# Two groups of small matmuls split by batch half over the rows of the array

## The reference

```python
state = np.zeros((B, H, D, D))                      # B, H, S, D = 4, 8, 768, 40
for t in range(S):
    y[:, :, t] = np.einsum('bhd,bhde->bhe', rt, state)
    Sa = np.einsum('bhde,bhe->bhd', state, at)
    state_decay = state * wt[:, :, None, :] - np.einsum('bhd,bhe->bhde', Sa, bt)
    state = state_decay + np.einsum('bhd,bhe->bhde', vt, kt)
...
h = x @ w_in                                        # then SoLU, layer norm, @ w_out
g = np.maximum(h, 0.0) + alpha * np.minimum(h, 0.0) # with h = x @ w_in of the second layer; then @ w_out
```

## Time and profile before

| | us |
|---|---|
| median of 3 runs | 997.64 |
| lowest and highest run | 991.07 and 1005.46 |
| the profiled execution's own time | 1002.32 |
| its span in the trace | 1000.5 |
| mean granted clock of TensorE in it | 0.974 |

### The profile page before, as it was taken

The page is one execution under the profiler, slowest core; times in us unless marked ns, Lnnn a source line. Parts: engine busy times, 40 slices in busy tenths (PEclk is TensorE's granted clock), DMA queues, the critical chain, the costliest instruction groups (busy, mean ns, idle before and its releaser), DMA issues.

```text
span 1000.5 us, 31301 instructions
## 1 busy us (share of the span) xinstructions
PE 919.4 (92%) x13248; PEld 872.5 (87%) x13248; DVE 655.5 (66%) x1135; ACT 438.2 (44%) x892; POOL 245.9 (25%) x453
## 2 busy tenths in 40 slices
PE   3479999989999989877999999999999999999997
PEld 3378998878899978776999999999999999999997
DVE  7967767767778855657655656575756556564734
ACT  3234454444445443246443535353534444353523
POOL 8676555745557540000000000000000000000000
PEclk9689999999999999998999999999999999999999
DMA  5735655565666553251010000000000000000000
GB/s 158 128 71 145 137 124 129 145 153 121 148 144 169 113 111 71 88 182 56 15 27 6 23 27 1 27 0 26 0 26 0 26 0 26 26 0 13 2 14 14
DMA packets 156813, 67.32 MB, mean 67 GB/s; under 512 B 120172, under 2 KB 146412, under 8 KB 156700
## 3 DMA queue, kind: packets, MB, share of 16 engines
q1 hardware_dynamic: 154588, 65.54, 27.5%
q10 hardware_dynamic: 2112, 0.13, 0.2%
HBM read 45.98 MB, written 19.66 MB: 66 GB/s over the span
## 4 chain that ended last, share of the span: by engine, by line
PE 63%; DVE 9%; POOL 8%; DMA 6%; issue 6%; SPq 4%; ACT 3%; DVEq 0%; ACTq 0%; POOLq 0%
PE acc L1104 6%; PE acc L1105 5%; PE acc L1106 5%; PE px L341 4%; PE mid L1104 4%; PE mid L1105 4%; PE mid L1106 4%; PE bank L1104 3%; PE bank L1106 3%; PE bank L1105 3%; POOL s_x L816 3%; POOL s_t L814 3%; SPq L232 3%; PE pq L402 2%; PE pa L310 2%
## 5 line engine op out<-in xcount | busy, mean ns | idle before, releaser
L1363 POOL TENSOR_TENSOR stats<-stats 128x1 f32<-128x1 f32 x24 | 13.2, 551 | 551.9 <-DVE stats L1425 551.9
L1450 DVE SCALAR_TENSOR_TENSOR stage<-mid,slopes 128x512 f32<-128x512 f32 x96 | 66.4, 691 | 107.7 <-ACT slopes L1291 107.7
L1104 PE MATMUL acc<-wo_h,act_h 128*128 128x320 f32 x384 | 122.0, 318 | 8.4 <-DVE act_l L1377 7.7
L1287 ACT ACTIVATE stage<-mid 128x512 f32<-128x512 f32 x96 | 57.1, 595 | 161.2 <-PE mid L1175 161.2
L1105 PE MATMUL acc<-wo_h,act_l 128*128 128x320 f32 x384 | 118.8, 309 | 0.0
L1106 PE MATMUL acc<-wo_l,act_h 128*128 128x320 f32 x384 | 118.5, 309 | 0.0
L1104 PE MATMUL mid<-zT_h,w_h 128*128 128x256 f32 x384 | 108.3, 282 | 7.6 <-DVE zT_l L1377 7.6
L1105 PE MATMUL mid<-zT_h,w_l 128*128 128x256 f32 x384 | 107.9, 281 | 0.0
L1106 PE MATMUL mid<-zT_l,w_h 128*128 128x256 f32 x384 | 107.5, 280 | 0.0
L793 POOL TENSOR_TENSOR al<-al,prod 40x512 f32<-40x512 f32 x48 | 70.8, 1475 | 101.7 <-DMA al<-a_features_first 89.2
L1291 ACT ACTIVATE slopes<-stage,minus_alpha 128x256 f32<-128x256 f32 x192 | 87.3, 502 | 3.1
(11 more groups left out here) (160 smaller groups left out, 2371.6 us busy)
## 6 DMA issues: line engine op xcount, KB each, us to landing
wkb<-wkb_features_first SPq DMA_DIRECT2D x46, 242.5 KB
rvu<-rv_features_first SPq DMA_DIRECT2D x48, 160.0 KB
l_scr<-lb SPq DMA_DIRECT2D x24, 256.0 KB, 4.4
x_scr<-x SPq DMA_DIRECT2D x24, 256.0 KB, 4.1
al<-a_features_first SPq DMA_DIRECT2D x48, 80.0 KB
sv<-v_time_first SPq DMA_DIRECT2D x48, 80.0 KB, 4.4
out<-y_sb SPq DMA_DIRECT2D x12, 320.0 KB, 2.2
d_scr<-s_x SPq DMA_DIRECT2D x12, 256.0 KB, 2.3
```

The source lines that it names most:

```text
L1104: pe.matmul(o, left[0], right[0], start=start, stop=False)
L1287: act.activation(neg[q % 2][:], mid[q % 2][:], ACT.Relu, scale=-1.0).then_inc(neg_ready, 1)
L1450: dve.scalar_tensor_tensor(out=act_f[q % 2][:], in0=mid[q % 2][:], scalar=0.0, in1=slope[q % 2][:], op0=ALU.max, op1=ALU.add).then_inc(act ...
```

## The change

Scores and read-outs are split by batch half. Each head has two matmuls in place of one: one with the rows of half 0, one with those of half 1, each with 128 stationary and 64 moving columns, and each half writes to a PSUM bank of its own (columns 0 to 511 and 512 to 1023). The moving operand of the scores is `al` itself; the tile `a_bd`, its copies on ScalarE and its zeroing go. `copy_l`, `mask_ka` and `mask_q` then work by half, over all 8 heads of a bank, and not by piece; the turns that ScalarE and VectorE took within a piece go. Scores are still issued in two parts of four heads, but all waits stand ahead of the first part, and l_done and q_done are raised once a group, behind the last matmul. The two PSUM banks that ScalarE cleared from `a_bd` at the start are cleared by VectorE.

```diff
@@ -202,7 +201,7 @@
                              rv_in[m, h].rearrange("e (h x) -> e h x", h=NH)).then_inc(rvu_loaded[m % 3], 16)
 
         def l_write(p):
-            sp.wait_ge(l_ready, 8 * p + 8)
+            sp.wait_ge(l_ready, 4 * p + 4)
             for h in range(2):
                 sp.dma_start(l_scr[p, :, h, 0:T * T].rearrange("l (s t) -> s l t", t=T),
                              lb[p % 3][HR[h]].rearrange("p g h t -> p (g h) t")).then_inc(l_out[p % 2], 16)
@@ -293,23 +292,26 @@
         save_y(NG - 1)
 
     def tensor(pe, beside):
-        def scores(m, piece):
-
-            pe.wait_ge(kbT_ready, m + 1)
-            pe.wait_ge(a_bd_ready, 2 * m + 2)
-            if m < AHEAD:
-                wait(pe, l_ready, 4 * (m - 2) + 4)
-                wait(pe, ka_ready, 4 * (m - 2) + 4)
-            else:
-                pe.wait_ge(kbn_ready, 2 * m - 1 + piece)
-            if m == AHEAD - 1:
-                pe.wait_ge(q_ready, 1 + piece)
+        def scores(m, part):
+
+            if part == 0:
+                pe.wait_ge(kbT_ready, m + 1)
+                pe.wait_ge(a_ready, 2 * m + 2)
+                if m < AHEAD:
+                    wait(pe, l_ready, 2 * (m - 2) + 2)
+                    wait(pe, ka_ready, 2 * (m - 2) + 2)
+                else:
+                    pe.wait_ge(kbn_ready, 2 * m)
+                if m == AHEAD - 1:
+                    pe.wait_ge(q_ready, 2)
             banks = score_banks(m)
-            for i in range(4):
-                h = piece * 4 + i
-                ins = pe.matmul(banks[:, h * P:(h + 1) * P], kbT[m % 3][:, h].rearrange("p a b -> p (a b)"),
-                                a_bd[:, :, h], start=True, stop=True)
-            ins.then_inc(l_done, 1)
+            for h in range(part * 4, part * 4 + 4):
+                for half in range(2):
+                    col = half * 512 + h * T
+                    ins = pe.matmul(banks[:, col:col + T], kbT[m % 3][ER[half], h].rearrange("p a b -> p (a b)"),
+                                    al[m % 7][ER[half], half, h], start=True, stop=True)
+            if part == 1:
+                ins.then_inc(l_done, 1)
 
         def turn_kb(m):
 
@@ -317,8 +319,8 @@
                 if m < AHEAD - 2:
                     wait(pe, kbn_ready, 2 * m - 1 + piece)
                 else:
-                    pe.wait_ge(l_ready, 4 * m + 2 + 2 * piece)
-                    pe.wait_ge(ka_ready, 4 * m + 2 + 2 * piece)
+                    pe.wait_ge(l_ready, 2 * m + 1 + piece)
+                    pe.wait_ge(ka_ready, 2 * m + 1 + piece)
                 bank = turn_bank(m, piece)
                 for i in range(4):
                     ins = pe.transpose(bank[:, i * P:(i + 1) * P],
...
@@ -387,21 +389,19 @@
         def read_out(m):
 
             pe.wait_ge(uT_ready, 2 * m + 2)
-            if m == 0:
-                pe.wait_ge(l_ready, 16)
-                pe.wait_ge(ka_ready, 16)
             pe.wait_ge(rvu_loaded[m % 3], use(m, 3, 32))
             if m == 0:
-                pe.wait_ge(l_ready, 16)
-                pe.wait_ge(ka_ready, 16)
+                pe.wait_ge(l_ready, 8)
+                pe.wait_ge(ka_ready, 8)
             if m == 1:
                 pe.wait_ge(kbn_ready, 2 * AHEAD)
-            for piece in range(2):
-                wait(pe, q_ready, 2 * m - 1 + piece)
-                for h in range(piece * 4, piece * 4 + 4):
-                    ins = pe.matmul(pq[:, h * P:(h + 1) * P], vuT[m % 3][:, h].rearrange("p a b -> p (a b)"),
-                                    rvu[m % 3][:, h, 0:4:3], start=True, stop=True)
-                ins.then_inc(q_done, 1)
+            wait(pe, q_ready, 2 * m)
+            for h in range(NH):
+                for half in range(2):
+                    col = half * 512 + h * T
+                    ins = pe.matmul(pq[:, col:col + T], vuT[m % 3][ER[half], h].rearrange("p a b -> p (a b)"),
+                                    r_bd[m % 3][half][ER[half], h], start=True, stop=True)
+            ins.then_inc(q_done, 1)
 
         def turn_state(m):
 
@@ -425,7 +425,7 @@
             for h in range(NH):
                 for half in range(2):
                     o = py[ER[half], h * T:(h + 1) * T]
-                    pe.matmul(o, kbn[m % 7][:, h, half], q[:, h, 1 - half], start=True, stop=False)
+                    pe.matmul(o, kbn[m % 7][:, h, half], q[:, h, half], start=True, stop=False)
                     ins = pe.matmul(o, sn[m % 3][:, h], r_bd[m % 3][half][:, h], start=False, stop=True)
             ins.then_inc(y_done, 1)
 
@@ -509,27 +509,21 @@
             dve.tensor_tensor(kbT[m % 3], kbT[m % 3], inv[:, :, 2:].unsqueeze(2).to_broadcast([P, NH, 2, T]),
                               ALU.mult).then_inc(kbT_ready, 1)
 
-        def mask_ka(m, piece):
-
-            dve.wait_ge(l_done, 2 * m + 1 + piece)
+        def mask_ka(m, half):
+
+            dve.wait_ge(l_done, m + 1)
             wait(dve, rhs_done, m - 6)
-            src = score_banks(m)[:, piece * 512:piece * 512 + 512].rearrange("p (n a t) -> p n a t", n=4, a=2)
-            for half in range(2):
-                other = HR[1 - half]
-                if m < AHEAD:
-                    dve.wait_ge(l_ready, 4 * m + 2 * piece + 2)
-                else:
-                    wait(dve, l_ready, half * (4 * m + 2 * piece + 1))
-                dve.tensor_tensor(al[m % 7][other, half, piece * 4:piece * 4 + 4], src[other, :, half],
-                                  repeated(later, other, 4), ALU.mult).then_inc(ka_ready, 1)
-
-        def mask_q(m, piece):
-
-            dve.wait_ge(q_done, 2 * m + 1 + piece)
+            other = HR[1 - half]
+            src = heads(score_banks(m)[:, half * 512:half * 512 + 512], NH, T)
+            dve.tensor_tensor(al[m % 7][other, half], src[other], repeated(later, other, NH), ALU.mult)\
+               .then_inc(ka_ready, 1)
+
+        def mask_q(m, half):
+
+            dve.wait_ge(q_done, m + 1)
             wait(dve, y_done, m)
-            dve.tensor_tensor(q[:, piece * 4:piece * 4 + 4].rearrange("p n a t -> p (n a) t"),
-                              pq[:, piece * 512:piece * 512 + 512].rearrange("p (n t) -> p n t", t=T),
-                              repeated(later, slice(0, P), 8), ALU.mult).then_inc(q_ready, 1)
+            dve.tensor_tensor(q[:, :, half], heads(pq[:, half * 512:half * 512 + 512], NH, T),
+                              repeated(later, slice(0, P), NH), ALU.mult).then_inc(q_ready, 1)
 
         def next_state(m):
 
@@ -600,10 +594,11 @@
             dve.memset(seeds[:], 0.0).then_inc(seeds_set, 1)
             dve.wait_ge(seeds_set, 1)
             dve.memset(seeds[:, :, 0:1], 1.0).then_inc(seeds_set, 1)
-            dve.memset(a_bd[:], 0.0).then_inc(a_bd_set, 1)
             dve.wait_ge(seeds_set, 2)
             front(0)
             front(1)
+            for z in (pu, py):
+                dve.memset(z[:], 0.0).then_inc(psum_set, 1)
             dve.wait_ge(masks_loaded, 16)
             mask_both(0)
             front(2)
@@ -663,16 +658,12 @@
         store_y(NG - 1)
 
     def scalar(act, beside):
-        def copy_l(m, piece):
-
-            act.wait_ge(l_done, 2 * m + 1 + piece)
+        def copy_l(m, half):
+
+            act.wait_ge(l_done, m + 1)
             wait(act, x_done, 4 * (m - 6) + 1)
-            src = score_banks(m)[:, piece * 512:piece * 512 + 512].rearrange("p (n a t) -> p n a t", n=4, a=2)
-            for half in range(2):
-                own = HR[half]
-                if m >= AHEAD:
-                    wait(act, ka_ready, half * (4 * m + 2 * piece + 1))
-                act.copy(lb[m // 2 % 3][own, m % 2, piece * 4:piece * 4 + 4], src[own, :, half]).then_inc(l_ready, 1)
+            src = heads(score_banks(m)[:, half * 512:half * 512 + 512], NH, T)
+            act.copy(lb[m // 2 % 3][HR[half], m % 2], src[HR[half]]).then_inc(l_ready, 1)
 
         def take_rhs(m):
             act.wait_ge(rhs_done, m + 1)
@@ -698,15 +689,6 @@
                 src = bank[:, 0:512].rearrange("p (n a w) -> p n a w", n=4, a=2)[:, :, :, 0:HD]
                 act.copy(kbn[m % 7][:, piece * 4:piece * 4 + 4], src).then_inc(kbn_ready, 1)
 
-        def spread_a(m):
-
-            if m == 0:
-                act.wait_ge(a_bd_set, 1)
-            act.wait_ge(a_ready, 2 * m + 2)
-            wait(act, l_done, 2 * m)
-            for half in range(2):
-                act.copy(a_bd[ER[half], half], al[m % 7][ER[half], half]).then_inc(a_bd_ready, 1)
-
         def d_read(p, blocks):
             act.wait_ge(dd_set, p + 1)
             act.wait_ge(d_out[p % 2], use(p, 2, 16))
@@ -729,21 +711,11 @@
                 act.copy(sv[(m + 2) % 3][ER[half], half], st[m % 2][ER[half]]).then_inc(sv_ready, 1)
 
         def prologue():
-            act.wait_ge(a_bd_set, 1)
-            act.copy(pu[:], a_bd[:, 0].rearrange("p h t -> p (h t)")).then_inc(psum_set, 1)
-            act.copy(py[:], a_bd[:, 0].rearrange("p h t -> p (h t)")).then_inc(psum_set, 1)
```

(17 more changed lines are left out.)

## The result

The changed kernel takes **1056.22 us** (median of 4 runs, 1050.64 to 1058.83) against 1000.88 in the comparison's runs of the kernel before: a ratio of 1.0559, interval [1.0464, 1.0655]. I had predicted 1023 with a range up to 1047: the direction was right, the time lies above the range. The profiled execution took 1058.83 us, 56.5 more than the one of before; its mean granted clock is 0.942 (0.974 before).

A forecast was written before the change was run, and what follows sets the result against it. TensorE's chain bounds the kernel, held back now and then by the GpSimd and SP loop. 29.2 + 1.05 - 14.4 - 1.7 + 8.8 = +22.9 on 1002.3 gives 1025; forecast 1023 us, between 1025 and 1020.5; range 1003 to 1047.

The forecast's parts named there:

- The wait that is added: Before Horner stage 3, TensorE waits for VectorE's mask and take_horner 2: 1.62 us in each of 18 steps, +29.2 us.
- The matmuls: Split scores and read-outs on TensorE cost the same as before: 0, bounds +0.6 and -0.4 us a step.
- Both rivals: Matmul halves run one after another, some 1100 us, chance 0.10; moving columns set the pace, 991 to 996 us, chance 0.12.
- What is given back: In steps 1 to 18, waits for late wkb loads go as TensorE's pair becomes slower than the loop: -14.4 us.
- the loop of GpSimd and SP: GpSimd's solve, then SP's scratch reads and wkb loads: 31.26 us a pair against 29.5 for two TensorE steps.
- The start: In the prologue, VectorE masks and scans earlier without waiting for ScalarE's copies: -1.7 us.
- The last masks: In steps 22 and 23, two masks instead of one behind the last read-out: +0.35 and +0.70, +1.05 us.
- The clock: TensorE's clock halves behind some of the new idle stretches: five falls of 1.75 us in 18 steps, +8.8 us.
- The rival that I did name: Clock falls in nearly every step: 1025 + 22, 1047 us; counted within the forecast's case, which has chance 0.78.
- M2: Theory from the experiments' expectations, not the prediction: split scores make TensorE's clock fall more readily behind a gap.

The follow-up runs named there:

- experiment 1: Changed kernel with VectorE's take_horner 2 moved ahead of both mask_ka masks: 1017.27 us, ratio 1.0148 to the kernel before.
- experiment 2: Kernel before, full matmuls, with the masks of both pieces waiting for the second scores piece from group 6 on: 1046.09 us, ratio 1.0478.
- experiment 8: Changed kernel with the scores' two parts cut by batch half instead of by heads, each raising l_done: 1069.2 us, ratio 1.0734.
- Experiment 9: wkb load for even steps issued earlier on SP, ahead of the solved blocks' read: 1016.2 us in the kernel before, 1016.81 us in the kernel of 7.
- experiment 5: Changed kernel with only four heads of the first mask ahead of take_horner 2, the rest behind it: 1045.45 us, ratio 1.0469.
- experiment 3: Changed kernel with the right side computed once more on TensorE between the scores' second part and Horner stage 3: 1034.29 us, ratio 1.0325.
- 7: Kernel of experiment 1 with the split matmuls on all 64 rows of a half instead of 40: 1010.65 us, ratio 1.0113.
- experiment 3b: Kernel of experiment 2, full matmuls and late masks, with the right side computed once more before Horner stage 3: 1027.97 us, ratio 1.0293.

## Why the prediction was wrong

**The wait that is added: right.** 1.62 us was predicted for each of 18 steps; the trace has 1.67, by the predicted chain of one mask, two takes and the hand-overs. Experiments 1 and 2 show that it comes from the order on VectorE and the late l_done alone.

**The matmuls: right.** 0 was predicted; read-outs are 0.05 us shorter, the two parts of the scores 0.08 together, 0.13 us a step. Both rivals fell. The halves run side by side; 2.00 against 1.04 us in experiment 8 shows what a part would have cost if not. The moving columns don't set the pace: half of them brought nothing. The Trainium skill, TensorEngine Tiling (Array Packing), says in its section Key Properties that different tiles can load weights and multiply at the same time, which 1.04 us agrees with; the twofold speed of its section Theoretical Speedup didn't come for 128 weight columns, with 1.93 us for 32 records against 1.98 for 16.

**What is given back: right.** 25.8 us of waits for wkb became 1.0. That the loop of GpSimd and SP stands behind them, as I argued from 31.26 us a pair, isn't settled. Experiment 9 fits it, since the loads issued earlier turn the wait into one for dd; but there the moved load itself delays the read of dd, by about as much as TensorE waits for it (six waits, 2.3 us at most).

**The start: wrong, small.** -1.7 was predicted, +1.8 came at uT of step 0. VectorE did get ahead, and its first solve with it, but the write of this solve to scratch took 3.9 us from its issue to the read behind it, and 2.3 before. Behind the read TensorE's next groups take longer, one of them 1.97 us where it took 1.15. The windows view gives a clock of 1.00 there, so why isn't settled. With the idle stretch and the longer fall of the clock in step 0, uT of step 1 is 5.2 late. The last masks: +1.05 predicted, 0.6 more in the last step; the last six steps together lost 4.3, with three falls of the clock in them (mean clock 0.89, and 0.98 before).

**The clock: the step that failed.** "I take five falls in 18 steps, +8.8; bounds 0 and 18 (+31.5)." The mechanism is the predicted one, but the term is mis-sized: five has no working behind it, and the clock fell in each of steps 1 to 17. A step of 18.29 us is 14.76 (the kernel before) - 0.13 + 1.67 + 1.99: the last is the clock, 17 x 1.99 = 33.8 us in steps 1 to 18 alone, where 8.8 was predicted. A short fall costs less than the 1.75 us that I took, 1.45 (steps of 17.75 us), but six of the falls were twice as long as the one that gave that price.

I had reasoned by the length of an idle stretch, from two with a fall and two without. The rows left out another stretch of the same trace: it is as long as the shorter of the two without a fall, a second of 0.62 us follows it closely, and behind them the clock fell (timeline, then windows):

```profile
374.80 0.57 PE L341 MATMUL px<-hh,lower 64*16 64x16 f32 x32 [1.25 <-DVE hh L560]
377.04 1.65 PE L365 MATMUL pr<-rhs,hh 64*64 64x40 f32 x32 [0.62 <-ACT rhs L680]
...
377.00:378.00 1.00, 0.96 (x24) 0.99 (x26) 0.36 (x1) 0.00 (x0) 0.34 (x2) 0.71 0.00 0
378.00:379.00 1.00, 1.00 (x24) 1.00 (x24) 0.00 (x0) 0.00 (x0) 0.00 (x0) 0.50 0.81 262
```

So lengths of 1.25 and 1.35 us were no ground for leaving falls out, and experiment 5 shows 17 falls in 17 steps with a stretch of 1.39 us. The rival that I did name, a fall in nearly every step, I priced at 22 us more than the forecast and set as the upper end of its case; it deserved to be its centre: 18 equal stretches, each as long as one that had led to a fall.

**The whole difference.** +22.9 was forecast for the profiled execution and 56.5 measured, 33.6 more: 23.7 in steps 1 to 18 (the clock 25.0 more, the wait 0.9 more, the matmuls 2.2 less), 5.3 up to uT of step 1, 4.6 behind step 18.

**By experiments:** of 55 us, 39 go with the order on VectorE (1). Of these at least 18 to 22 are falls of the clock (3, where the path is as long as with the stretch), the rest is the stretch itself, 18 x 1.67 = 30, less what else fills a step once it is gone. The remaining 10 to 15 us (1, 7) stay open, and M2 with them: shown is only that the split scores alone bring some 7 of them, that the split read-outs alone bring none, and that falls of the clock in the start and the last six steps, and behind stretches that the profile doesn't explain, hold part of it.

## What to carry to other kernels

When several rises of a semaphore are merged into the last, look at the waiting engine's queue: what stands behind the wait there, and which engine needs that, decides the cost, and moving one instruction ahead of the wait can take most of it back (39 of 55 us here). Price an idle stretch on TensorE's path with the half clock that may follow it, here 2 us for 1.7, and if the stretch repeats in every step, with a fall each time. Halving the moving columns brought nothing here, where the weight columns stayed at 128.

## What was not expected of the hardware

- The clock falls with no idle stretch (experiment 8: 25.00 of 25 us busy, 0.80 to 0.93), where some 4 us of each step go to matmuls on one side of the array one after another. Alternating between the sides, with the same matmuls, it mostly didn't (experiment 1: 4 falls in 17 steps).
- The length of one idle stretch doesn't tell whether the clock falls: behind 1.39 us it did 17 times in 17 (experiment 5), behind 1.72 us 14 times in 18 (experiment 2), behind 1.35 us in the kernel before not the earlier trace rows, behind 0.66 us in experiment 3b not once in steps 1 to 17, behind 0.61 us with split scores (experiment 3) five times in 17.
- With the turns between them gone, ScalarE and VectorE read the same PSUM bank at the same time, each its half of the partitions (both start at 302.60 in the changed kernel). VectorE's mask takes 0.69 us, what its other operation of 512 elements takes in the earlier trace rows, and ScalarE's copy 0.58.
